# A third buffer for the q and k loads of an attention stage, and its unit loops written out

## The reference

```python
out_d = sm_attn(q_d, k_d, v_d)              # q_d, k_d, v_d: means over 4 positions
mask = np.abs(pos[:, None] - pos[None, :]) < factor          # factor = 4
scores = np.where(mask, scale * np.matmul(q, k.transpose(0, 1, 3, 2)), -1000000000.0)
return np.repeat(out_d, factor, axis=2) + softmax(scores) @ v
```

## Time and profile before

| | us |
|---|---|
| median of 3 runs (830.36 to 832.86) | 832.72 |
| the profiled execution, its own time | 831.72 |
| its span | 829.9 |
| PE busy in the span | 803.5 |
| DVE, ACT, POOL busy | 652.5, 521.6, 201.3 |

### The profile page before, as it was taken

One profiled execution on the slowest core, in us unless ns is written; L12 is line 12 of the kernel. 1 busy time (PEld: TensorE's weight loads), 2 busy tenths in 40 slices (PEclk: granted clock), 3 DMA queues, 4 the chain that ended last, 5 costly groups with the idle time before them and its releaser, 6 DMA issues.

```text
span 829.9 us, 15752 instructions
## 1 busy us (share of the span) xinstructions
PE 803.5 (97%) x5787; PEld 776.1 (94%) x5787; DVE 652.5 (79%) x945; ACT 521.6 (63%) x816; POOL 201.3 (24%) x207
## 2 busy tenths in 40 slices
PE   7988889999989999999999999999999999999998
PEld 4766679999989999999999999999999999999997
DVE  6889867989998867888867888899755677665465
ACT  4766656568646577746577655687455777465763
POOL 6889876612024512035400000000000000000000
PEclk9999999999999999999999999999999999999999
DMA  6777758767768797768787777877887778877773
GB/s 204 222 211 199 207 153 290 245 212 269 254 219 274 239 320 265 261 219 265 252 293 253 242 244 252 276 241 243 289 281 253 274 254 267 279 260 265 260 269 126
DMA packets 98315, 205.42 MB, mean 248 GB/s; under 512 B 8416, under 2 KB 56032, under 8 KB 98240
## 3 DMA queue, kind: packets, MB, share of 16 engines
q1 hardware_dynamic: 98240, 204.42, 75.0%
HBM read 160.87 MB, written 43.52 MB: 246 GB/s over the span
## 4 chain that ended last, share of the span: by engine, by line
PE 78%; POOL 9%; DVE 7%; issue 3%; DMA 2%; ACT 0%; SPq 0%; POOLq 0%; DVEq 0%; ACTq 0%
PE hid L309 41%; PE yp L332 36%; POOL vpair L895 3%; DVE gr L482 2%; DMA vn<-in_v 2%; POOL pband L898 2%; POOL G L920 2%; DVE wh L284 1%; POOL pavg L902 1%; POOL vavg L908 1%; DVE xs L245 1%; DMA sums_in<-G 1%; POOL G L918 1%; PE pt L1080 0%; POOL G L924 0%
## 5 line engine op out<-in xcount | busy, mean ns | idle before, releaser
L309 PE MATMUL hid<-xs,wh 128*128 128x384 f32 x2016 | 352.0, 334 | 2.7 <-DVE G L469 1.1
L309 PEld LDWEIGHTS hid<-xs,wh 128*128 128x128 f32 x2016 | 349.2, 188 | 4.7 <-issue 4.6
L332 PE MATMUL yp<-gr,wh 128*128 128x384 f32 x2016 | 350.9, 334 | 1.7 <-DVE gr L482 1.7
L332 PEld LDWEIGHTS yp<-gr,wh 128*128 128x128 f32 x2016 | 349.4, 188 | 2.2 <-issue 2.2
L275 ACT ACTIVATE wh<-wr 128x1024 fp32r<-128x1024 f32 (+1 forms) x164 | 164.6, 1003 | 154.4 <-PE hid L309 115.7
L482 DVE TENSOR_TENSOR gr<-G,gr 128x768 fp32r<-128x768 f32 x144 | 138.5, 971 | 48.3 <-ACT gr L382 48.3
L382 ACT ACTIVATE gr<-G 128x768 fp32r<-128x768 f32 x144 | 121.8, 846 | 68.9 <-PE yp L332 64.8
L284 DVE TENSOR_TENSOR wh<-wr,wh 128x1024 fp32r<-128x1024 f32 x76 | 89.6, 1180 | 21.7 <-ACT wh L275 21.7
L349 ACT ACTIVATE G<-G 128x1152 f32<-128x1152 f32 x48 | 55.8, 1162 | 0.0
L457 DVE TENSOR_TENSOR hv<-p,hid 128x384 f32<-128x384 f32 x48 | 26.4, 549 | 27.6 <-PE hid L309 19.5
L472 DVE TENSOR_TENSOR G<-hv,hid 128x384 f32<-128x384 f32 x48 | 26.4, 551 | 26.2 <-PE hid L309 26.1
(11 more groups left out here) (90 smaller groups left out, 772.3 us busy)
## 6 DMA issues: line engine op xcount, KB each, us to landing
wh<-rests SPq DMA_DIRECT2D x72, 512.0 KB, 3.8
wr<-sums_out SPq DMA_DIRECT2D x48, 512.0 KB, 5.0
wr<-in_w_out SPq DMA_DIRECT2D x36, 512.0 KB, 5.4
rests<-wh SPq DMA_DIRECT2D x36, 512.0 KB, 3.4
wr<-sums_in SPq DMA_DIRECT2D x40, 384.0 KB, 4.0
wr<-in_w_in SPq DMA_DIRECT2D x40, 256.0 KB, 3.5
qk<-in_qkT SPq DMA_DIRECT2D x16, 576.0 KB, 5.9
G<-in_w_in SPq DMA_DIRECT2D x12, 512.0 KB, 6.5
```

The source lines that it names most:

```text
L309: last = eng.matmul(hid[:, at, 0:HALF], lhsT=wh[:, w % SLOTS, part, a % 4, cc * P:(cc + 1) * P], rhs=xs[:, rest, q, cc, :], start=start an ...
L332: last = eng.matmul(yp[:, at + m, 0:HALF], lhsT=wh[:, w % SLOTS, part, p % 4, m * P:(m + 1) * P], rhs=gr[:, p, rest, :], start=start and p ...
```

## The change

A third place for q and k is made from the first 1152 of the 1792 numbers per partition of the tile `wt`. Unit n uses place n mod 3, each place with its own semaphore. At the start SP asks for q and k of unit 2 as well, between the two loads of `vwin`; in `body(u)` it asks, at the same point and behind the same waits, for those of u+3. All loops are gone: every unit is written out, on every engine, with constant addresses. `early`, which the looped units skipped, is now called for units 1 and 2 too; it has nothing to do there.

```diff
-    EARLY = 3
...
-            qk = sb("qk", [P, 2, 2, S])
+            two = sb("qk", [P, 2, 2, S])
+
+            qk = [two[:, 0], two[:, 1], ffn.wt[:].rearrange("p a n -> p (a n)")[:, 0:2 * S].rearrange(
+                "p (i s) -> p i s", i=2)]
...
-        qk_in = [sem(f"qk_in{i}") for i in range(2)]
+        qk_in = [sem(f"qk_in{i}") for i in range(3)]
...
-            with eng.Fori(0, (EARLY - 1) // 2) as m:
-                body(Unit(m, 1), False, False)
-                body(Unit(m + 1, 0), False, False)
-            for n in range(EARLY, UNITS - 1):
+            for n in range(1, UNITS - 1):
                 body(Unit(n // 2, n % 2), False, False)
...
-                eng.dma_start(qk[:, u.odd, :, :], src).then_inc(qk_in[u.odd], DMA_INC)
+                eng.dma_start(qk[u.n % 3], src).then_inc(qk_in[u.n % 3], DMA_INC)
...
                 load_vwin(u)
+                load_qk(u.after().after())
                 load_vwin(u.after())
...
-                if not isinstance(u.n, int) or u.n + 2 < UNITS:
+                if u.n + 3 < UNITS:
...
                         eng.wait_ge(band_sc, 2 * (u.n + 1))
                         eng.wait_ge(qk_sum, u.n + 1)
-                    load_qk(u.after().after())
+                    load_qk(u.after().after().after())
...
-            with eng.Fori(0, (UNITS - 4) // 2) as m:
-                body(Unit(m, 1))
-                body(Unit(m + 1, 0))
-            for n in range(UNITS - 3, UNITS):
+            for n in range(1, UNITS):
                 body(Unit(n // 2, n % 2))
...
-                eng.wait_ge(qk_in[u.odd], DMA_INC * (u.half + 1))
-                eng.tensor_reduce(sums4[:], qk[:, u.odd, :, :].rearrange(
+                eng.wait_ge(qk_in[u.n % 3], DMA_INC * (u.n // 3 + 1))
+                eng.tensor_reduce(sums4[:], qk[u.n % 3].rearrange(
```

More of the change, by code:

```diff
@@ L822, in start @@
                 load_vwin(u)
+                load_qk(u.after().after())
                 load_vwin(u.after())
             def body(u, first=False):
-                if not isinstance(u.n, int) or u.n + 1 < UNITS:
+                if u.n + 1 < UNITS:
                     eng.wait_ge(v_half, u.n + 1)
                     load_vn(u.after())
-                if not isinstance(u.n, int) or u.n + 2 < UNITS:
+                if u.n + 3 < UNITS:
                     if first:
@@ L841, in body @@
                         load_vwin(u.after())
-                if u.odd and (not isinstance(u.n, int) or u.n + 1 < UNITS):
+                if u.odd and u.n + 1 < UNITS:
                     eng.wait_ge(ffn.w0_sum, 2 * u.n)
@@ L976, in body @@
                                    scale=1.0 / FACTOR).then_inc(oavg_cp, 1)
-                if not first and isinstance(u.n, int):
+                if not first:
                     early(u.n)
@@ L1098, in head_scores @@
                     return eng.matmul(sc[half, bank, (t - a) * WIN:(t - a + 1) * WIN],
-                                      lhsT=qk[rows, u.odd, 0, t * QT:(t + 1) * QT],
-                                      rhs=qk[rows, u.odd, 1, starts[t]:starts[t] + WIN],
+                                      lhsT=qk[u.n % 3][rows, 0, t * QT:(t + 1) * QT],
+                                      rhs=qk[u.n % 3][rows, 1, starts[t]:starts[t] + WIN],
                                       start=False, stop=t in (LEFT - 1, NT - 1), skip_group_check=True)
```

## The result

Over 12 executions of each the changed kernel takes 830.79 us (median, 828.56 to 831.50), the kernel before 833.53 us (830.36 to 838.72). The ratio is 0.996, 95% interval 0.9944 to 0.9977: 3.3 us, 0.4%, faster (the medians differ by 2.7 us). The profiled execution took 831.09 us, span 829.3; the spans of the two profiled executions differ by 0.6 us only (829.9 before), because that of the kernel before took 831.72 us, 1.8 us under its median. So the gain rests on the repeated runs, and the profiles show where time moved, in one execution before and two after. Run again later beside other kernels, the changed kernel stood at 0.9951 (0.9935 to 0.9966) of the kernel before, 830.17 us, and its second profile has the same shape.

A forecast was written before the change was run, and what follows sets the result against it. No attention-stage engine was full, so the chain of waits, nearly all GpSimd's, counted. Terms -5.6 + 1.8 + 0 - 0.6 = -4.4 us took 831.72 to 827.3; with a median of 828.3, it said 828.0, range 824.3 to 831.3.

The forecast's parts named there:

- The q and k waits go (-5.6 us): Attention units 2 to 15: all VectorE waits for q and k vanish, gaining 5.6 us, bounds 2 and 7.4.
- the 1.8 us forecast: Attention units: the part of GpSimd's 7.4 us `rca` waits that is VectorE's own work and stays, 1.8 us.
- A wait for `vn` in four short legs (+1.8): Units 5, 7, 11, 13: single-place `vn` is waited for again, 1.8 us lost, bounds 0 and 3.0.
- The stretching stays at 12.2 us: Attention units: GpSimd's stretching beside VectorE's early pieces is only shifted, not removed, and left at 12.2 us.
- The rule on the port pair: GpSimd and VectorE overlaps: skill says first starter keeps the lock; forecast followed the trace, GpSimd losing either way; no size.
- The extra load at the start (0): Start: second `vwin` and first `G` come 1.5 us later, `G` at 14.1; nothing taken, 0.4 us lost at half rate.
- A `pband` late by over 0.5 us: Start of the attention stage: the first `pband` late by this much would show the forecast wrong.
- The loops (-0.6): SP's queue: written-out addresses issue `G` 0.7 us and `vn` about 0.1 us sooner, gaining 0.6 us, bounds 0 and 2.
- The second stage unchanged: Feed-forward stage, PE 99% busy: the change touches nothing there; a change of more than 1 us would show it wrong.
- Rival 1: Attention units: `vn` stays in time and VectorE catches up, 8.0 us gained, 824; chance 0.17.
- Rival 2: Attention units: the single `vn` place takes most of the gain, leaving 1.1 us, 831.3; chance 0.15.
- Rivals 3 and 4: Later `vn` landings slow units, 837, chance 0.05; q and k weren't what L1008 awaited, time stays 832.5, chance 0.05.

The follow-up runs named there:

- the third experiment: Changed kernel with the extra first load of q and k issued last at the start, behind second `vwin` and first `G`: 830.33 us, ratio 0.9969.
- the combined one: Changed kernel with `G` issued behind `vn`, extra first load last at the start, 13 extra matmuls in PE's start pauses: 829.46 us, ratio 0.9949.

## Why the prediction was right, and where its steps failed

The direction came out, and the mechanism of the gain: VectorE no longer waits for q and k, and GpSimd no longer for `rca` behind it. The size came out smaller: forecast 828.0 against 832.72, -4.7 us; measured -3.3 by the ratio and -2.7 by the medians, 830.79 us, inside the range of 824.3 to 831.3. For the 13 units the forecast was -4.4 us, and the two profiles show -3.55 and -3.95. That this sum came so near is in part luck, since a wait that did not come stood in it in place of stretching and waits for `G` that did. By its own steps:

- **The q and k waits go (-5.6 us): right.** Between units 2 and 15 all of VectorE's are gone, and GpSimd's waits for `rca` fell from 7.4 us to the 1.8 us forecast (2.0 in the second profile).
- **A wait for `vn` in four short legs (+1.8): wrong as a mechanism, near in size by luck.** No wait for `vn` is left there in the changed kernel. Of the four legs named, 6.07 us each before, two grew: that of unit 5 to 6.79 through stretching, that of unit 13 to 7.39 through a wait for `G` of 1.17 us and stretching (6.13 in the second profile); those of units 7 and 11 stayed at 6.08. `G`, which I had only counted as something to clear the queue, is waited for with 1.3 us (2.1 in the second profile). With `G` first, `vn` waits 3.1 us at the place where `G` was late in the second profile. That suggests one limit under two names, but does not show it.
- **The stretching stays at 12.2 us: mis-sized by 2.5 us.** By the same reckoning it is 84.35 - 13 x 5.36 = 14.7 us after and 12.2 before (13.2 in the second profile); with the early pieces moved away it is near 1 (the reckoning's own error, no operation is stretched). Why it grows is not shown: 12 operations of GpSimd are stretched before and after, each beside one of VectorE's pieces, and they are stretched by more.
- **The rule on the port pair: I was wrong to go by the earlier trace rows.** With only the loops written out, VectorE's L245 takes 2.02 us behind an earlier `vpair`, and in four more profiles 2.02 to 2.03 us. So it is not always GpSimd that loses. This agrees with what the Trainium skill says ("SBUF — State Buffer", section "SBUF: two separate sides"): the holder keeps the pair for its instruction and the other blocks. L920 and L284 in rows 4 and 5 still disagree, by their recorded starts, with the rule that the one that starts first keeps it.
- **The extra load at the start (0): nearly right.** `G` landed at 14.5 against 14.1 reckoned; 0.53 us of wait (0.9 in the second profile). No cost of it can be told, as the third experiment says.
- **Not in the sum at all: the start (+1.1 us).** A `pband` late by over 0.5 us was one of the forecast's own signs of being wrong; unit 2's is. The clock falls in the start in both kernels, and in both profiles of the changed one it stays down for some 6.8 us. Filling PE's pauses kept it up and brought unit 2 forward by 2.07 us. What makes the low stretch long or short is open: it is as long with `G` first, and short (3.4 us) in two versions with exactly the changed kernel's start, so it is not fixed by the change. With the low stretch short unit 2 is late all the same (24.49 to 24.60), so what costs the 1.1 us stays open too.
- **The loops (-0.6): the size fits, the reason does not.** I priced them through `vn`, which is not waited for. Written out alone they give 0.9999; the third place without them 0.9987; side by side the third place is 2.1 us faster with them than without. The 0.7 us that `G` is issued earlier is a likely reason, since GpSimd waits 6.8 us for `G` in the profile with the loops kept, but that is the slowest execution of its kernel, and no run isolates it.
- **The second stage unchanged: off by 1.9 us in the first profile**, 1.1 in the second. A change of more than 1 us there was another of the forecast's signs of being wrong. But versions with the same second stage take 714.0 to 717.3 us from unit 15 on, where the changed kernel has 716.2 and 715.5 and the kernel before 714.4 in its one profile. So the profiles don't tell whether the change moves it.

Rival 1 (no wait for `vn`) was right on the wait and wrong on the time. Rival 2 (the gain is taken by the next limit) was wrong on `vn` and on the size, but a weaker form of it is what the forecast missed. Rivals 3 and 4 did not come about.

## What to carry to other kernels

When a wait is removed in a stage where three engines are each 90% busy, ask what each of the others does with the time: here 5.8 us of waits for `rca` gone gave 3.55 us in the stage, and removing every remaining DMA wait gave 0.75 us more, in one profile. Time ahead bought for one load suggests putting the loads that now have slack behind those that have none; here that removed the wait for `G`, but its gain in time was not resolved. Look at the granted clock in 2 us stretches before reckoning with PE's durations in a stage with pauses. And before a wait is put down to a fall of the clock, look which came first: here a VectorE piece stretched by 1 us, GpSimd's wait for it and PE's pause stood in front of the fall.

## What the runs showed of the hardware

- In six of the twelve new profiles (loops written out, third place with loops, fillings, no later q and k, the combined one, early pieces last) PE's granted clock fell to 0.5 somewhere inside the attention stage, between units 2 and 15, for some 3.4 us each time (twice in that with loops). VectorE then waited for PE, 0.93 us in the combined kernel and 1.35 us with the loops written out. In the combined kernel and in that without later q and k the fall came after pauses of PE of 1.98 and 1.99 us in front of the transposes. The second profile of the changed kernel has a pause of 2.34 us at that place and that with a second place for `vn` one of 1.98 us, both without a fall, and the version with fillings at the start has a fall after one of 1.56 us: the single pause does not decide.
- Where an early piece of VectorE and an operation of GpSimd overlap, either can be the one that is stretched: in the changed kernel L920 1.89 us for 0.73, with only the loops written out L245 2.02 us for 0.95. A stretched L245 of 2.02 to 2.03 us stands in five of the twelve new profiles, each time behind L256 at unit 9 (once at unit 10 too), and each time `pband` waits 1.87 or 1.88 us for `rcb` after it.
